# Retention attention and two expert layers on one core: loads, the first weight splits, the gate logits and the last output rows rearranged

## The reference

```python
def _attn_ref(q, k, v):                    # batch 2, heads 8, seq 768, head_dim 64
    for t in range(S):
        state = gamma * state + einsum('bhd,bhe->bhde', k[:, :, t], v[:, :, t])
        y[:, :, t] = scale * einsum('bhd,bhde->bhe', q[:, :, t], state)

def _moe_ref(x, w_gate, w1, w2):           # x (1536, 512), 8 experts, hidden 1024
    P = exp(x @ w_gate - max)
    for _ in range(8):                     # rows, then columns, are normalised
        P /= P.sum(1, keepdims=True) + 1e-09
        P /= P.sum(0, keepdims=True) + 1e-09
        P *= N / E
    for e in range(E):
        out += P[:, e:e + 1] * (maximum(x @ w1[e], 0) @ w2[e])
```

## Time and profile before

| | us |
|---|---|
| median of 3 runs | 1560.71 |
| profiled execution, whole | 1563.57 |
| its span, first to last instruction | 1561.8 |
| PE busy | 1548.5 (99%) |
| PE weight load busy | 1405.0 (90%) |
| DVE busy | 881.9 (56%) |
| ACT busy | 445.8 (29%) |
| POOL busy | 53.3 (3%) |
| data moved | 67.28 MB |

### The profile page before, as it was taken

One profiled execution on the slowest core, in us unless ns is written; L12 is line 12 of the kernel. 1 busy time (PEld: TensorE's weight loads), 2 busy tenths in 40 slices (PEclk: granted clock), 3 DMA queues, 4 the chain that ended last, 5 costly groups with the idle time before them and its releaser, 6 DMA issues.

```text
span 1561.8 us, 21255 instructions
## 1 busy us (share of the span) xinstructions
PE 1548.5 (99%) x8228; PEld 1405.0 (90%) x8228; DVE 881.9 (56%) x1434; ACT 445.8 (29%) x860; POOL 53.3 (3%) x45
## 2 busy tenths in 40 slices
PE   8999999999999999999999999999999999999999
PEld 7888998899889988998999899988998899889988
DVE  5846756546545555464555554667555546455553
ACT  4421322223213222232133122333322223213321
POOL 4400000000000000000000000012000000000000
PEclk9999999999999999999999999999999999999999
DMA  9201001011010010010110100101001011011011
GB/s 318 98 0 55 27 28 55 3 52 55 1 54 30 23 54 26 27 54 0 54 54 0 54 27 28 55 0 55 29 26 55 19 36 54 0 54 54 1 43 66
DMA packets 34699, 67.28 MB, mean 43 GB/s; under 512 B 2256, under 2 KB 2384, under 8 KB 34640
## 3 DMA queue, kind: packets, MB, share of 16 engines
q1 hardware_dynamic: 34064, 66.16, 12.2%
q10 hardware_dynamic: 576, 0.30, 0.1%
HBM read 63.31 MB, written 3.15 MB: 43 GB/s over the span
## 4 chain that ended last, share of the span: by engine, by line
PE 97%; DMA 1%; DVE 1%; ACT 0%; SPq 0%; issue 0%; POOL 0%; DVEq 0%; POOLq 0%
PE bank L1066 17%; PE bank L1065 17%; PE bank L1064 17%; PE bank L1043 15%; PE bank L1047 15%; PE bank L1045 15%; DMA qt_in<-in_q_t 1%; PE bank L926 1%; PE bank L964 1%; DMA k_in<-in_k 0%; PE bank L946 0%; PE bank L1011 0%; PE bank L958 0%; DVE w_lo L625 0%; PE bank L992 0%; PE bank L994 0%
## 5 line engine op out<-in xcount | busy, mean ns | idle before, releaser
L1043 PE MATMUL bank<-x_hi,w_hi 128*128 128x384 f32 x1344 | 450.5, 335 | 4.2 <-DVE w_lo L625 2.3
L1047 PE MATMUL bank<-x_hi,w_lo 128*128 128x384 f32 x1344 | 450.2, 335 | 0.0
L1045 PE MATMUL bank<-x_lo,w_hi 128*128 128x384 f32 x1344 | 450.0, 335 | 0.0
L1066 PE MATMUL bank<-w_hi,h_lo 128*128 128x512 f32 x1152 | 449.2, 390 | 0.0
L1065 PE MATMUL bank<-w_lo,h_hi 128*128 128x512 f32 x1152 | 449.0, 390 | 0.0
L1064 PE MATMUL bank<-w_hi,h_hi 128*128 128x512 f32 x1152 | 448.5, 389 | 0.0
L789 DVE SCALAR_TENSOR_TENSOR acc<-bank,gate,acc 128x512 f32<-128x512 f32 x252 | 189.2, 751 | 374.7 <-PE bank L1066 374.7
L490 ACT COPY ups<-bank 128x384 f32<-128x384 f32 x288 | 138.0, 480 | 908.3 <-PE bank L1047 908.3
L742 DVE TENSOR_TENSOR ups<-bank,ups 128x384 f32<-128x384 f32 x288 | 155.3, 554 | 189.5 <-ACT ups L490 167.8
L1043 PEld LDWEIGHTS bank<-x_hi,w_hi 128*128 128x128 f32 x1344 | 252.9, 188 | 6.9 <-issue 2.6
L1066 PEld LDWEIGHTS bank<-w_hi,h_lo 128*128 128x128 f32 x1152 | 216.2, 188 | 45.0
(11 more groups left out here) (83 smaller groups left out, 503.0 us busy)
## 6 DMA issues: line engine op xcount, KB each, us to landing
w_raw<-in_moe_w SPq DMA_DIRECT2D x47, 1024.0 KB, 5.1
kt_in<-in_k_t SPq DMA_DIRECT2D x12, 256.0 KB, 3.7
qt_in<-in_q_t SPq DMA_DIRECT2D x12, 256.0 KB, 5.8
v_in<-in_v SPq DMA_DIRECT2D x12, 256.0 KB, 6.2
k_in<-in_k SPq DMA_DIRECT2D x10, 256.0 KB, 6.7
out<-acc SPq DMA_DIRECT2D x2, 768.0 KB, 3.5
out<-acc SPq DMA_DIRECT2D x6, 256.0 KB, 2.0
w_first<-in_moe_w SPq DMA_DIRECT2D x1, 1024.0 KB, 5.1
```

Of the source, the lines that this page charges most:

```text
L1043: nc.tensor.matmul(o, w1_hi[:, w, kc, fs], x_hi[:, x, kc, at], start=start and kc == 0, stop=False, skip_group_check=True)
L1045: nc.tensor.matmul(o, w1_hi[:, w, kc, fs], x_lo[:, x, kc, at], start=False, stop=False, skip_group_check=True)
L1047: last = nc.tensor.matmul(o, w1_lo[:, w, kc, fs], x_hi[:, x, kc, at], start=False, stop=kc == 1, skip_group_check=True)
L1066: last = nc.tensor.matmul(o, h_lo[:, f, b, rows], w2_hi[:, f, :], start=False, stop=(n == UC - 1))
```

## The change

Seven edits, all in the order or the shape of work at the ends of the program and at the seam.

1. **Loads.** SP loads the keys and values of a step together with its queries, not one step later; `rise` moves from ACT's queue to SP's; the first w1 comes in four DMAs of 256 KB, one behind each of the steps 5 to 8, not as one of 1 MB behind step 7.
2. **Warm-up.** Three more warm-up matmuls stand behind the first score and three behind the second.
3. **First weight splits.** a11, S2 with S3, and S1 are split by instructions of their own, written ahead of those for the last token sums. `a11_ready` alone releases the first product. POOL forms S3 ahead of `raise_q(10)`, S1 and S2 between it and `raise_q(11)`, and S4 behind.
4. **Gate weights.** They are split at the start of the program, into a layout (1024 columns, two batches in rows 0 to 15 and 64 to 79) with which both batches' logits land in one bank: 32 matmuls, 2 copies of 80 rows, 6 transposes of 80 rows.
5. **Row sums** of the second layer's probabilities move from before the first w2 split to behind `down(2, 1)`.
6. **Seam.** PE's wait for the last row of `acc` ahead of `up(L1_LAST + 1, 0)` is removed; the same condition is waited for before that `up`'s second product, where the transposes stand.
7. **Last row.** The last row of 128 tokens is computed in two halves of 256 columns, each with its own bank half, addition and store.

```diff
@@ block.sync
             load_qk(0, 0)
+            load_k(0, 0)
             sp.dma_start(mask[:, :, :, :], ...).then_inc(mask_in, 16)
+            load_v(0, 0)
             for s in range(1, STEPS):
-                if s == 8:
-                    load_w1(moe_w1, 0, 0)
+                if s == 2:
+                    sp.dma_start(rise[1][:, :, :], ...).then_inc(rise_in, 16)
                 if c > 1:
                     sp.wait_ge(y_done, s - 4 + 1)
                 load_qk(c, b)
-                load_kv((s - 1) // BATCH, (s - 1) % BATCH)
-            load_kv(CH - 1, 1)
+                load_kv(c, b)
+                if 5 <= s < 5 + DC:
+                    at = slice((s - 5) * P, (s - 4) * P)
+                    sp.dma_start(w1_raw[:, s - 5, :], moe_w1[0, at, 0:UF]).then_inc(w1_first, 16)
...
+            for half in range(2):
+                sp.wait_ge(acc_written, downs_before(last, 1) + (2 * CPB + half))
+                at = slice(half * DM // 2, (half + 1) * DM // 2)
+                sp.dma_start(out_d[:, row, at], acc[:, row, at]).then_inc(stored, 16)
@@ block.gpsimd
-            first_w1_sums()
+            first_w1_sum(0)
+            raise_q(STEPS - 2)
+            first_w1_sum(1)
+            first_w1_sum(2)
+            raise_q(STEPS - 1)
+            first_w1_sum(3)
@@ block.scalar
+            gate_weights()
             for s in range(STEPS):
                 if s == STEPS - 1:
-                    split_w1_high(0, 0, first=True)
+                    first_w1_high(1)
+                    first_w1_high(2)
...
+                if s == STEPS - 3:
+                    first_w1_high(0)
@@ block.vector
             mask_scores(0)
+            dve.wait_ge(wg_hi_ready, 1)
+            low(wg_parts[:, :, 64 + E1:64 + 2 * E1], wg_raw[:, :, :], wg_parts[:, :, 64:64 + E1])
+            low(wg_parts[:, :, P + E1:P + 2 * E1], wg_raw[:, :, :], wg_parts[:, :, P:P + E1]).then_inc(wg_lo_ready, 1)
...
+                if s == STEPS - 2:
+                    first_w1_low(0)
+                if s == STEPS - 1:
+                    first_w1_low(1)
+                    first_w1_low(2)
...
-            split_w1_low(0, 0)
-            split_w1_low(0, 1)
@@ block.tensor
+            def warm(n):
+                for i in range(n):
+                    nc.tensor.matmul(bank[7][:, 0:P], state[1][:, 0, :], state[1][:, 0, :], start=True, stop=True)
...
             score(0)
+            warm(WARM_GAP)
             for s in range(STEPS):
                 if s < STEPS - 1:
                     score(s + 1)
+                if s == 0:
+                    warm(WARM_GAP)
                 attend(s)
...
+                parts = [(0, X_B11, 64), (2, X_B21, P), (0, X_T1, 0), (2, X_B22, 0)]
                 for p in range(PAIRS):
...
+                    if p == 1:
+                        pe.wait_ge(h_ready, 4)
+                    for n, (c, m, w) in enumerate(parts):
+                        for kc in range(2):
+                            nc.tensor.matmul(ps_logit[p][:, 0:BLK], wg_parts[:, c + kc, w:w + P],
+                                             x_hi[:, m, kc, at], start=(n == 0 and kc == 0), stop=False)
...
             x_split(CH + CPB)
-            pe.wait_ge(acc_written, downs_before(L1_LAST, 1) + 2 * CPB)
             up(L1_LAST + 1, 0, x2=CPB)
...
+                    for half in range(2):
+                        pe.wait_ge(acc_written, downs_before(k, p) + (2 * CPB - 2 + half))
+                        o, at = half_bank(half), slice(half * DM // 2, (half + 1) * DM // 2)
+                        for f in range(UC):
+                            nc.tensor.matmul(o, h_hi[:, f, 0, rows], w2_hi[:, f, at], start=(f == 0), stop=False)
...
```

More of the change, by code:

```diff
@@ L218, in row_of, with half_bank @@
             return (CH if u < CPB else 0) + CPB * p + u % CPB
+        def half_bank(half):
+            return down_bank[1 - half][:, half * DM // 2:(half + 1) * DM // 2]
         def up_psum(kind, half):
@@ L353, in _ @@
             decay_k(1)
[L354 to L364, removed]
-                nc.gpsimd.tensor_tensor(s2, a21, a11, ALU.subtract).then_inc(w1_summed, 1)
-                pool.wait_ge(w1_summed, 3)
-                nc.gpsimd.tensor_tensor(s4, a12, s2, ALU.subtract).then_inc(w1_summed, 1)
-            for s in range(BATCH, STEPS - 1):
-                raise_q(s)
-                if s < STEPS - BATCH:
-                    decay_k(s)
-            first_w1_sums()
+            for s in range(BATCH, STEPS - BATCH):
+                raise_q(s)
+                decay_k(s)
+            first_w1_sum(0)
[4 more added lines that the diff above has]
+            first_w1_sum(3)
             sums_low(CH - 1)
@@ L900, in _ @@
             hidden(L2_LAST, 1)
-            down(L2_LAST, 1, gate2, E2 - 1)
+            for u in range(2 * CPB - 1):
+                add_expert(L2_LAST, 1, u, gate2, E2 - 1, "add")
+            i = row_of(1, 2 * CPB - 1)
+            dve.wait_ge(acc_written, downs_before(L2_LAST, 1) + (2 * CPB - 12))
+            for half in range(2):
+                a = acc[:, i, half * DM // 2:(half + 1) * DM // 2]
+                dve.wait_ge(down_done, downs_before(L2_LAST, 1) + (2 * CPB + half))
+                nc.vector.scalar_tensor_tensor(a, half_bank(half), gate2[:, i, E2 - 1:E2], a,
+                                               ALU.mult, ALU.add).then_inc(acc_written, 1)
         @block.tensor
@@ L967, in attend @@
                 last.then_inc(y_done, 1)
+            def warm(n):
+                for i in range(n):
+                    nc.tensor.matmul(bank[7][:, 0:P], state[1][:, 0, :], state[1][:, 0, :], start=True, stop=True)
             pe.wait_ge(zeroed, 4)
-            for i in range(WARM):
-                nc.tensor.matmul(bank[7][:, 0:P], state[0][:, 0, :], state[0][:, 0, :], start=True, stop=True)
+            warm(WARM)
             score(0)
+            warm(WARM_GAP)
             for s in range(STEPS):
@@ L1017, in up @@
                 for n, (w, x, kind, start) in enumerate(PRODUCTS):
-                    if p == 0:
+                    if p == 0 and not first:
                         pe.wait_ge(w1_ready, 4 * k + {W_A11: 1, W_S1: 1, W_S2: 2, W_S3: 2, W_S4: 3}.get(w, 4))
+                    elif first and n == 0:
+                        pe.wait_ge(a11_ready, 1)
+                    elif first:
+                        pe.wait_ge(w1_ready, {W_S2: 1, W_S3: 1, W_S1: 2, W_S4: 3}.get(w, 4))
                     if n == 1 and x2 is not None:
@@ L1072, in down @@
                         transpose_x2(x2 + 2)
+                if last_rows:
+                    rows = slice((CPB - 1) * P, CPB * P)
+                    for half in range(2):
+                        pe.wait_ge(acc_written, downs_before(k, p) + (2 * CPB - 2 + half))
+                        o, at = half_bank(half), slice(half * DM // 2, (half + 1) * DM // 2)
+                        for f in range(UC):
+                            nc.tensor.matmul(o, h_hi[:, f, 0, rows], w2_hi[:, f, at], start=(f == 0), stop=False)
+                            nc.tensor.matmul(o, h_hi[:, f, 0, rows], w2_lo[:, f, at], start=False, stop=False)
+                            last = nc.tensor.matmul(o, h_lo[:, f, 0, rows], w2_hi[:, f, at],
+                                                    start=False, stop=(f == UC - 1))
+                        last.then_inc(down_done, 1)
             def unit(k):
@@ L1111, in _ @@
             unit(L2_LAST - 1)
-            unit(L2_LAST)
+            up(L2_LAST, 0)
+            down(L2_LAST, 0)
+            up(L2_LAST, 1)
+            down(L2_LAST, 1, last_rows=True)
 def _constants():
```

138 lines of the change are left out of this document (87 added, 51 removed).

## The result

| | before | after |
|---|---|---|
| median, us | 1561.13 (1558.86 to 1562.22, 6 runs) | 1552.68 (1552.39 to 1553.43, 6 runs) |
| ratio, 95% interval | | 0.995 (0.9939 to 0.9961) |
| profiled execution, whole / span | 1563.57 / 1561.8 | 1552.96 / 1551.2 |

A forecast was written before the change was run, and what follows sets the result against it. PE makes 97% of the chain, so only its waits, clock falls and matmul columns count. 1.07 + 1.64 - 0.15 + 3.3 + 1.39 + 0.2 + 1.0 + 0 = 8.5 us, 1560.7 to 1552.2; range 1549.0 to 1557.0.

The forecast's parts named there:

- Start of attention: Start of the kernel: with the new load order `attend(2)` starts at 16.84 instead of 17.91, gain 1.07 us, low end -0.64.
- The clock at the start: Between 7.87 and 11.28 PE's idle time falls from 1.63 to some 0.9 us and the clock holds at 2.4 GHz.
- Load wait of step 8: Attention, step 8: w1 in quarters removes PE's wait for queries, gain 1.64 us, ends 0 and 1.64.
- the rival of 1.06 us a unit: Slow load queue with w1 mixed in: load waits and clock falls make the kernel slower, 1566 us; chance 0.05.
- End of attention: Last `attend`: POOL's added sums ahead of `raise_q(11)` delay it by 0.15 us, ends 0 and 0.9.
- First `up`: First `up`: no gap or clock fall, seventh product waits for DVE's sum; 3.3 us taken, from between 3.4 and 4.9.
- Logits 1.39, gates 0.2: Gate logits: 32 matmuls instead of 40 gain 1.39 us; six wider transposes instead of 12 gain 0.2, ends 0 and 0.4.
- Seam 1.0: Seam between the layers: PE's wait for the last row of `acc` goes, gain 1.0 us, low end 0.
- Last row 0: End of the program: more matmul time against a shorter last addition, gain 0, ends -0.25 and +0.15 us.
- the clock falls all the same: Start of attention: warm-ups fill only part of the wait, the term is -0.64, time 1554.0 us; chance 0.17.
- A load wait left in step 8: Attention: load wait remains in part and `raise_q(11)` is 0.9 late, gain 6.1 us; chance 0.15, alone or with clock fall.
- nothing that counts: Quarters of w1 late, a11 waits for the fourth, clock falls at 55 again: gain 1.1, time 1559.6 us; chance 0.08.

The follow-up runs named there:

- the old start: After with before's load order (`rise` on ACT's queue, keys and values one step later) and no gap warm-ups, w1 still in quarters: 1551.54 us, ratio to before 0.9942.

## Why the prediction was right or wrong

The forecast, 1552.2, and its sign were right. One step failed, two terms were too small, and the errors met: that the total came within 0.5 us is in part luck.

- **Start of attention: the step that failed.** The times that it worked out for the new order held to 0.1 us: 9.77 for the second score (9.69), 11.68 for `attend(0)` (11.65), 16.84 for `attend(2)` (16.88, or 16.95 in the chain). What failed is what they were held against. "`attend(2)` starts at 16.84 instead of 17.91" took the one profiled execution for the kernel; two others start it at 15.20 and 15.36, and the old order of loads in the new kernel at 15.25. The term is not +1.07 but -1.5 to -1.7, as the old start confirmed (1.4 us in the whole time). The loads put ahead of the second queries cost nearly all of that. The warm-ups cost 0.16, and the early fall against which they stand was in one of three profiles of before and in none of ten runs of the new kernel with the old order. The ends given, 1.07 and -0.64, did not hold it, since both were counted from the same execution.
- **The clock at the start.** It held, but not for the reason given. PE was to idle 0.9 us between 7.87 and 11.28, not 1.63; in after's profile it idled 1.66, and the clock stayed up all the same. The wait for the second queries had grown as the first score ended earlier. What decides between a fall and none in that stretch stays open.
- **Load wait of step 8.** Gone, as forecast, and the load of the earlier trace rows with it. But it was 1.3 and 0.7 in the other profiles, so the term is 0.7 to 1.6. With the old start spreading w1 takes all of it away; with after's later start a part of it would have gone anyway, and spreading gives 0.3 to 0.6. The queue kept its pace, and of the rival of 1.06 us a unit nothing was seen.
- **End of attention.** 0.15 was taken, 0.14 measured: `attend(11)` stands 1.23 behind L1019, which is 1.09 without a wait.
- **First `up`.** 3.3 was taken from ends of 3.4 and 4.9, and 4.3 came. The mechanism was right in its parts: the first product started without a gap, and POOL's low part stopped the copies of w2 (3.50 us for 1.30; POOL itself took 3.03, not 2.40). DVE's sum was put at 66.7 in the old time, 64.1 in after's; it came at 63.12, and the stall was 2.2 us, not 2.4. Most of the missing microsecond is in the count of DVE's row: 1.21 was added for the low part of the token sums and 0.60 taken off for a11, though both stand between the last masks and the first hidden sum in the old order as well as in the new. Without these two the sum would have been put 0.6 sooner. So the wait before the seventh product was 0.44, not 1 to 2. The Trainium skill ("GPSIMD Engine Reference", Specifications) says that POOL contends with DVE instructions that have two SBUF inputs and with those in a two-port mode. The low parts that met POOL's operation, 4.56 us for 2.35, agree with the first half. The copies have one input, and their stall agrees with the second, but that they run in such a mode no row shows. Moving POOL's operation away brought the copies back to 1.28. Of the 4.3, 1.6 is the clock, and that only in executions in which it fell there.
- **Logits 1.39, gates 0.2.** 1.5 for the logits, and 0.48 for the gates: a transpose of 80 rows took 0.06 us, no more than one of 16.
- **Seam 1.0.** 1.2 in the profiles, and the wait came back when it was undone.
- **Last row 0.** The 24 matmuls took 2.88 us, as worked out from the two widths. The last addition is 0.27 shorter, as worked out too. What was left out is the last store: it is half the size, and the program ends 2.15 us behind the last addition, not 2.46. Together it is about 0.5, above the high end given (0.15).

Against the more typical execution of before (span 1558.8) the terms are -1.7 + 1.3 - 0.15 + 4.3 + 1.5 + 0.5 + 1.2 + 0.5 = 7.5, and the spans differ by 7.6. Against the one with no fall at all (before with gap warm-ups, 1557.5) it is 6.3. From the forecast's 8.5 to 7.5 the way is -2.8 for the start, -0.3 for the load wait, +1.0 for the first `up`, +0.4 for logits and gates, +0.2 and +0.5 for seam and last row. So a total that is 1 us off hides an error of 3 one way and of 2 the other. The measured gain is 8.45 by the first medians and 7.2 by the last ones (1560.15 and 1552.98). The 2.9 us by which the profile of before lay above the median were taken off at the end as if no term hung on them, when they were a fall of the clock and late loads that the start and the load wait counted as gains.

Of the rivals, "the clock falls all the same" did not happen in any of 11 runs. A load wait left in step 8, the slow load queue and "nothing that counts" are ruled out by the waits.

## What to carry to other kernels

When the profiled execution is slower than the median of the runs, find out first what it has that the others don't, and leave that out of every term: a term that is won from a disturbance of one execution is no gain. Compare the mean clocks of all runs, not one profile, before a warm-up or a gap is judged. And at a start bound by loads, count what each load put ahead delays; here the order "all of step 0 first" cost 1.4 to 1.5 us, though the only wait that it lengthened was that of the second score.

## What the runs showed of the hardware that I had not expected

- The same program falls to the lower clock in some executions and not in others: 0 to 3 times a run in the 50 runs of before, by their mean clocks. An idle time of 2.3 us at the first `up` brought a fall in three profiles of four; one of 1.6 us there, the 1.64 us of before in step 8 and after's 1.66 us at 9.69 brought none. Where the third fall of three runs lies is open.
- A copy (CAST) on DVE is held up by a two-input operation of POOL like a two-input one: 3.50 us for 1.30, where the low parts took 4.56 for 2.35; POOL's own took 3.03 and 2.94 for 2.40.
- Loads at the start landed up to 1.1 us apart between executions of the same program (`attend(0)` at 11.08, 10.01 and 10.19).
